# Delta rule: the state summed in PSUM and block-diagonal over both row halves, small row tiles for the other products, y turned by an identity

## The reference

```python
# attention by the delta rule: batch 4, heads 8, 768 tokens, head dim 48
k_n = k / (np.linalg.norm(k, axis=-1, keepdims=True) + 1e-06)
for t in range(S):
    y[:, :, t] = np.einsum('bhd,bhde->bhe', q[:, :, t], state)
    v_old = np.einsum('bhde,bhd->bhe', state, kt)
    state = state + bt * np.einsum('bhd,bhe->bhde', kt, vt - v_old)
# then two feed-forward layers over 3072 tokens, d_model 384, d_ff 2048
g = (a0 + a1*h + a2*h2 + a3*h3) / (1 + |b0|*|h| + |b1|*h2 + 1e-6)      # layer 1
g = h * tanh(softplus(h))                                            # layer 2
```

## Time and profile before

| | us |
|---|---|
| median of 3 runs | 1184.11 |
| lowest, highest | 1168.52, 1193.58 |
| the profiled execution | 1173.33 |
| its span, first to last instruction | 1171.5 |

### The profile page before, as it was taken

The page is one execution under the profiler, slowest core; times in us unless marked ns, Lnnn a source line. Parts: engine busy times, 40 slices in busy tenths (PEclk is TensorE's granted clock), DMA queues, the critical chain, the costliest instruction groups (busy, mean ns, idle before and its releaser), DMA issues.

```text
span 1171.5 us, 22278 instructions
## 1 busy us (share of the span) xinstructions
PE 1071.8 (91%) x9321; PEld 870.6 (74%) x9366; DVE 950.9 (81%) x1045; ACT 766.7 (65%) x1039; POOL 171.6 (15%) x328
## 2 busy tenths in 40 slices
PE   5388999999888899999999999889999999999997
PEld 3276877877766677787787777668888888888885
DVE  4965567554569999999999999999887888878785
ACT  1535456466367687777867768687676767667664
POOL 2088787780000000000000000000000000000000
PEclk7588889996899999999999999999999999999999
DMA  7625447343021010000101003230010101010000
GB/s 198 185 62 159 137 111 192 97 110 124 22 87 54 1 55 1 25 30 0 54 0 54 1 1 108 81 107 28 1 55 1 54 0 54 1 54 1 25 4 27
DMA packets 30489, 69.03 MB, mean 59 GB/s; under 512 B 4160, under 2 KB 11840, under 8 KB 30400
## 3 DMA queue, kind: packets, MB, share of 16 engines
q1 hardware_dynamic: 30144, 66.98, 19.2%
q10 hardware_dynamic: 256, 0.79, 0.3%
HBM read 53.60 MB, written 14.16 MB: 58 GB/s over the span
## 4 chain that ended last, share of the span: by engine, by line
DVE 35%; PE 33%; issue 3%; ACT 2%; DVEq 0%; ACTq 0%
PE o_ps L837 6%; PE o_ps L838 5%; PE o_ps L839 5%; PE h_ps L837 5%; PE h_ps L839 5%; PE h_ps L838 5%; DVE val L1022 5%; DVE val L1041 5%; DVE val L1054 5%; DVE g_lo L1060 5%; DVE den L1014 5%; DVE den L1049 5%; DVE pa L1020 4%; PE h_ps L881 0%; ACT den L901 0%
## 5 line engine op out<-in xcount | busy, mean ns | idle before, releaser
L910 ACT ACTIVATE g_hi<-val 128x1024 fp32r<-128x1024 f32 x96 | 102.0, 1062 | 99.7 <-DVE val L1054 93.6
L837 PE MATMUL o_ps<-g_hi,w_hi_late 128*128 128x512 f32 x288 | 116.8, 405 | 20.5 <-DVE g_lo L1060 20.4
L837 PE MATMUL o_ps<-g_hi,w_hi_early 128*128 128x512 f32 x288 | 114.8, 399 | 14.3 <-ACT stage L947 9.2
L1054 DVE SCALAR_TENSOR_TENSOR val<-den,val 128x1024 f32<-128x1024 f32 x96 | 117.7, 1226 | 10.7 <-DVE den L1049 0.5
L1060 DVE SCALAR_TENSOR_TENSOR g_lo<-val,g_hi 128x1024 fp32r<-128x1024 f32 x96 | 117.6, 1225 | 1.6 <-ACT g_hi L910 1.5
L837 PE MATMUL h_ps<-x_hi,w_hi_early 128*128 128x512 f32 x288 | 112.2, 390 | 2.0 <-DVE val L1022 2.0
L837 PE MATMUL h_ps<-x_hi,w_hi_late 128*128 128x512 f32 x288 | 112.5, 391 | 1.6 <-DVE w_lo_late L88 1.6
L838 PE MATMUL o_ps<-g_lo,w_hi_late 128*128 128x512 f32 x288 | 113.8, 395 | 0.0
L839 PE MATMUL o_ps<-g_hi,w_lo_early 128*128 128x512 f32 x288 | 113.5, 394 | 0.0
L838 PE MATMUL o_ps<-g_lo,w_hi_early 128*128 128x512 f32 x288 | 113.4, 394 | 0.0
L839 PE MATMUL o_ps<-g_hi,w_lo_late 128*128 128x512 f32 x288 | 113.3, 393 | 0.0
(11 more groups left out here) (111 smaller groups left out, 2360.2 us busy)
## 6 DMA issues: line engine op xcount, KB each, us to landing
w_raw<-w SPq DMA_DIRECT2D x16, 768.0 KB, 6.1
kv_run<-kv_n SPq DMA_DIRECT2D x24, 384.0 KB, 4.6
x_raw<-x_dram SPq DMA_DIRECT2D x12, 768.0 KB, 5.8
kq_run<-kq_t SPq DMA_DIRECT2D x44, 192.0 KB, 3.5
kq_gram<-kq_t SPq DMA_DIRECT2D x40, 192.0 KB, 6.7
x_dram<-stage SPq DMA_DIRECT2D x24, 192.0 KB, 4.0
x_dram<-stage SPq DMA_DIRECT2D x6, 768.0 KB, 4.3
out<-stage SPq DMA_DIRECT2D x5, 768.0 KB, 4.1
```

The source lines that it names most:

```text
L837: nc.tensor.matmul(dst, hi, rhs_hi, start=first, stop=False)
L910: act_fn(g_hi[:, n % 2], val[:, n % 2], ACT.Copy, scale=-1.0).then_inc(g_hi_ready, 1)
L1054: dve_stt(val[:, e], den[:, e], 2.0, val[:, e], ALU.subtract, ALU.mult).then_inc(g_ready, 1)
```

## The change

- **State.** It is no longer added up by DVE in SBUF. `update` adds in PSUM over the whole kernel (a start flag only for the first two steps), and the sum is copied to `state` after each step: the low row half by DVE (`copy_low`), the high by ACT (`copy_high`). `state` is block-diagonal over the two row halves, with zeros elsewhere.
- **k and q products.** Both use all 128 rows with 32 columns and 96 moving: 8 products each where there were 16. k and q of a turn are loaded once, into a ring of three turns, where they were loaded twice; the unused partitions are zeroed by POOL and, for turn 0, loaded by eight more transfers on ACT's queue (`load_pads`).
- **`solve` and `within`.** 16 products each of 32 rows, 32 columns and 48 moving, one for each head and batch, straight from `x_mat` and `p_mat`. `x_blk`, `p_blk` and `u_row` and the instructions that fill them go.
- **y.** It comes out by token; ACT copies it (`copy_y`), PE turns it with two products with an identity (`turn_y`, 96 columns, 128 moving) one step later, ACT copies it again (`copy_turned`).
- **keep_warm.** The two products in each step go. The burst of 12 stands ahead of every turn (before: turns 0 and 1), and PE waits ahead of it for that turn's inverse.
- **Order.** `weights(1)` moves behind the first inverse; `squares(tau + 3)` stands at s = 1 of turn tau on ACT, where squares(tau + 4) stood in chunk 2; `root_inverse` moves from s = 7 to s = 4; `turn_x` is always at s = 7.

```diff
-WARM = 2
-        kq_gram = sb("kq_gram", [P, CT, 2, G2 * V * B, C])
-        kq_run = sb("kq_run", [P, CT, 2, G2 * V * B, C])
+        kq = sb("kq", [P, RING * CT, 2, G2 * V * B, C])
...
+        def load_pads(q, c):
+            n = 2 * G2 * V * B * C
+            for r in range(HALVES):
+                q.dma_start(kq[64 * r + D:64 * r + 64, slot(0, c)].rearrange("p a s t -> p (a s t)"),
+                            kq_t[0, r][0:64 - D, c * n:(c + 1) * n]).then_inc(pads_loaded, 16)
...
             def k_state(tau, c, g):
-                pe.wait_ge(state_ready, q + 1)
+                pe.wait_ge(low_ready, q + 1)
+                if q >= 2:
+                    pe.wait_ge(high_ready, q - 1)
                 by_event()
-                for u, r, v in slots:
+                for v in range(V):
                     for b in range(B):
-                        s = B * v + b
-                        last = nc.tensor.matmul(ks_ps[quad(b), r, D * v:D * v + D],
-                                                kq_run[rows(r), c, 0, B * V * g + s],
-                                                state[rows(r), g, D * s:D * s + D], start=True, stop=True)
+                        at = HALVES * D * v
+                        last = nc.tensor.matmul(ks_ps[quad(b), at:at + HALVES * D],
+                                                kq[:, slot(tau, c), 0, B * (V * g + v) + b],
+                                                state[:, g, v, b].rearrange("p r d -> p (r d)"), start=True, stop=True)
...
             def solve(tau, c, g):
                 for u in range(U):
-                    last = nc.tensor.matmul(hz_ps[:, u], x_blk[:, c, U * g + u], z[:, g, u],
-                                            start=True, stop=True)
+                    for b in range(B):
+                        last = nc.tensor.matmul(hz_ps[quad(b), D * u:D * u + D],
+                                                x_mat[quad(b), tau % 2, HEADS * c + U * g + u],
+                                                z[quad(b), g, u], start=True, stop=True)
...
             def within(tau, c, g):
+                pe.wait_ge(q_done, q + 1)
+                by_event()
+                for v in range(V):
+                    for r in range(HALVES):
+                        for b in range(B):
+                            at = D * (HALVES * v + r)
+                            last = nc.tensor.matmul(y_bank[g][quad(b), at:at + D],
+                                                    p_mat[quad(b), tau % RING, HEADS * c + U * g + V * r + v],
+                                                    u_blk[quad(b), g, V * r + v, b],
+                                                    start=False, stop=True, skip_group_check=True)
+
+            def turn_y(q):
+                pe.wait_ge(y_copied, q + 1)
...
+                for r in range(HALVES):
+                    last = nc.tensor.matmul(turn_ps[0:V * D, P * r:P * r + P], y_tok[:, q % 2, r], ident[:],
+                                            start=True, stop=True)
...
             for tau in range(T):
                 for s in range(NQ):
...
-                    elif (tau, s) == (1, 0):
-                        pe.wait_ge(gram_used, 4 * (tau + 2))
-                        pe.wait_ge(inv_ready, 1)
+                    if tau and s == 0:
+                        pe.wait_ge(inv_ready, tau)
+                        if tau + 1 < T:
+                            pe.wait_ge(gram_used, 4 * (tau + 1) + 4)
                         by_event()
                         keep_warm(BURST)
-                    elif gram:
-                        pe.wait_ge(gram_used, 4 * (tau + 2) + fill)
-                        keep_warm(WARM)
                     solve(tau, c, g)
-                    if gram:
+                    if tau + 2 < T and 0 <= fill < 4:
                         gram_fill(tau + 2, fill)
                     q_state(tau, c, g)
...
+                    if q:
+                        turn_y(q - 1)
                     update(tau, c, g)
                     within(tau, c, g)
...
         def _(act):
+                    if q:
+                        copy_turned(q - 1)
+                    copy_high(tau, c, g)
+                    copy_y(tau, c, g)
+                    if c + 1 < CT:
+                        scale_v(tau, c + 1, g)
                     elif tau + 1 < T:
+                        scale_v(tau + 1, 0, g)
+                    if s == 1 and tau + 3 < T:
+                        squares(tau + 3)
...
         def _(dve):
-                dve_tt(u_row[:, g, 0:U * D].rearrange("p (u d) -> p u d", u=U), hz_ps,
-                       wgt[:, tau, cg:cg + U].unsqueeze(2).broadcast_to([P, U, D]), ALU.mult).then_inc(u_ready, 1)
-            def add_state(tau, c, g):
-                own = state[:, g, 0:V * B * D]
-                dve_tt(own, own, st_bank[g][:, 0:V * B * D], ALU.add).then_inc(state_ready, 1)
+            def copy_low(tau, c, g):
+                dve.wait_ge(st_done, index(tau, c, g) + 1)
+                nc.vector.tensor_copy(state[rows(0), g, :, :, 0], st_ps[g][rows(0)]).then_inc(low_ready, 1)
```

More of the change, by code:

```diff
@@ L188, in index, with slot, fill_of, bank_of @@
             return NQ * tau + G2 * c + g
-        slots = [(V * r + v, r, v) for v in range(V) for r in range(HALVES)]
+        def slot(j, c):
+            return CT * (j % RING) + c
+        def fill_of(bank):
+            return bank.rearrange("p (a c g v k) -> p a c g v k", a=2, c=2, g=G2, v=V)
+        def bank_of(j, f):
+            return early_banks[4 * j + f] if j < 2 else side_ps[:]
         STEPS = 2 * (C - 1)
-        def substitute(eng, tt, j, own, step, done):
-            for r in range(C - 1, 0, -1):
+        def rounds(eng, tt, j, own, step, done, first, last):
+            for r in range(first, last, -1):
                 shape = [P, r, C - r]
@@ L352, in gram_fill @@
                         for b in range(B):
-                            kq = operands[rows(r), 2 * cp + c2, :, B * s + b, :]
-                            last = nc.tensor.matmul(fill[quad(b), :, c2, s // V, s % V], kq[:, 0], kq,
+                            both = kq[rows(r), slot(j, 2 * cp + c2), :, B * s + b, :]
+                            last = nc.tensor.matmul(fill[quad(b), :, c2, s // V, s % V], both[:, 0], both,
                                                     start=True, stop=True)
                 last.then_inc(gram_done, 1)
-            def keep_warm(n):
-                for _ in range(n):
-                    nc.tensor.matmul(gram_bank[:], busy[:, 0:P], busy, start=True, stop=True)
             def k_state(tau, c, g):
@@ L455, in _ @@
                         k_state(tau + 1, 0, 0)
-                    if not gram:
-                        if tau + 2 < T and fill == 4:
-                            pe.wait_ge(gram_used, 4 * (tau + 2) + 4)
-                        keep_warm(WARM)
+                    if q:
+                        turn_y(q - 1)
                     update(tau, c, g)
                     within(tau, c, g)
+            turn_y(NQ * T - 1)
         @block.scalar
@@ new lines, in copy_high, with copy_turned @@
+            def copy_high(tau, c, g):
+                act.wait_ge(st_done, index(tau, c, g) + 1)
+                nc.scalar.activation(state[rows(1), g, :, :, 1], st_ps[g][rows(1)], ACT.Copy).then_inc(high_ready, 1)
+            def copy_turned(q):
+                tau, c, g = q // NQ, q % NQ // G2, q % G2
+                if c % 2 == 0 and g == 0:
+                    act.wait_ge(hand.y_stored[c // 2], 16 * tau + 16)
+                act.wait_ge(t_done, q + 1)
+                nc.scalar.activation(y_stage[0:V * D, :, g, P * c:P * c + P],
+                                     turn_ps[0:V * D, 0:HALVES * P].rearrange("p (r n) -> p r n", r=HALVES),
+                                     ACT.Copy).then_inc(t_copied, 1)
@@ L724, in _ @@
                         scale_gram(tau + 2, fill)
-                    add_state(tau, c, g)
+                    if s == (5 if tau == 0 else 4) and tau + 3 < T:
+                        root_inverse(tau + 3)
+                    copy_low(tau, c, g)
                     if (tau, s) == (0, 0):
```

357 lines of the change are left out of this document (160 added, 197 removed).

## The result

The changed kernel takes 1151.5 us (median of four runs, 1149.3 to 1156.6); the kernel before, beside it, 1176.3 (1168.1 to 1193.6). The ratio is 0.986, with a 95% interval of 0.982 to 0.991: faster by 1.4%, which the bound of 2% calls the same. The ratio is taken over fast runs alone, so it lies nearer to 1 than the quotient of the two medians, 0.979. The forecast was 1145 us, with a range of 1127 to 1185 and a chance of 0.64 for faster by more than 2%, 0.22 for a result in between. The profiled execution of the changed kernel is the slowest of its four, 1156.6 us (span 1154.8); that of before took 1173.3, so the two traces differ by 17 us where the medians differ by 25.

What follows compares the result with a forecast made beforehand. PE's own products were taken as the bound, with the clock and POOL setting the loop's end. Turns summed to an end at 291 us instead of 319.9: 29 less, 0.6 back, 1173.3 - 28 = 1145 us; range 1127 to 1185.

Steps and rivals of the forecast that it cites:

- 20 steps and 8 gram fills at 1.2 GHz: Turn 0, and turns 1 and 2 after two warm steps, at low clock: 4.8 us a step, 1.9 a fill.
- The step: One warm step of the loop: PE products of 2.35 us in sum, 2.8 us taken for it; bounds 2.5 and 3.3.
- priced: PE products: a record costs (2P + N) cycles of 2.4 GHz divided by tiles used in turn; good to about 20%.
- waits for PE to pass: Each step: more waits on PE (`y_copied`, `t_copied`, `q_done`, two for the state), the reason given for taking 2.8 us.
- Row tiles overlap: solve and within: four row tiles work at once, 11.7 ns a record, 0.37 us each; 47 ns without overlap.
- ACT's wait for squares: Turns 1 and 2: `squares(tau+3)` comes some 2.5 us late, PE stalls, and the rest of those turns runs at 1.2 GHz.
- Turn lengths: Six turns of the loop: 46 us for turn 0, 48 each for 1 and 2, then 31.6, 28 and 30; end at 291.
- POOL: Inverses on POOL: periods of 38.1 us, the last inverse ready at 261 us, ahead of turn 5.
- The clock staying low for lack of keep_warm: Rival, chance 0.15: without keep_warm the clock falls soon after each burst; loop ends at 354, 1208 us.
- Handovers that cost half a microsecond more: Rival, chance 0.15: waits PE meets with nothing queued make a warm step 3.3 us; loop ends at 312, 1167 us.
- Row tiles that take turns: Rival, chance 0.05: solve and within take 1.5 us each, a step 5.1; loop ends at about 349, 1203 us.
- POOL as the only bound: Rival, chance 0.20: the clock holds through most turns and each ends waiting for the inverse; loop ends at 279, 1133 us.

Runs made afterwards that it cites:

- wide kernel: Changed kernel with solve and within each as four products of 128 rows by 128 columns, computing something else; 1145.2 us, ratio to before 0.974.
- seventh: Changed kernel with turn_y in three column tiles of 32 instead of one of 96; 1154.9 us, ratio to before 0.989.
- eighth: Changed kernel with both turn_y and update in column tiles of 32; 1160.7 us, ratio to before 0.990.
- sixth: Changed kernel with squares(tau + 4) and its load moved back to chunk 2 of turn tau; 1151.9 us, ratio to before 0.987.
- third: Changed kernel with keep_warm's two products put back into each step; 1157.4 us, ratio to before 0.989.
- fourth: Changed kernel with the burst of 12 products only ahead of turn 0, the waits kept; 1152.2 us, ratio to before 0.982.
- the shifted one: Changed kernel with 128 events of PE's sequencer, no array work, added in the prologue; 1155.5 us, one run.

## Where the prediction was right and where it failed

**The number (partly luck).** The forecast of 1145 is 6.5 us under the median, and two errors stand against each other in it. It put 20 steps and 8 gram fills at 1.2 GHz, 111 us; a mean clock of 0.89 over 245 us comes to some 54 us at that level. And it put nothing for the supply of instructions, which stopped PE for 37 us inside groups.

**The step (right).** 2.35 us of products plus something for handovers gave 2.8; measured 3.02. The pieces: solve 0.45 from start to start (priced 0.37 without the border), q_state 0.35 (0.27), k_state 0.45 (0.27), turn_y 0.60 (0.53), update 0.81 (0.54), within 0.36 (0.37). What is over, 0.67 us, is not "waits for PE to pass" as the prediction had it but changes of the tile's shape. There are four in a step: solve to q_state 170 ns, k_state to turn_y 255, turn_y to update 309, update to within 415, where two groups of one shape follow each other in 22. The price goes with the moving columns of the product ahead of the change (48, 96, 128 and 192) and not with the shape that follows: behind update it is 415 ns with solve, within or the wide within next, and in the kernel before within (128 moving) to solve takes the same 309. The tile ahead counts as well: behind a solve of 128x128 tiles, 48 moving, it is 246 in the wide kernel and 247 in the kernel before, not 170. The seventh and eighth kernels take two of these away by making the shapes equal. By the Trainium skill (TensorEngine Tiling (Array Packing), Key Properties) a change of the tiling mode drains the array; the traces agree, and give the size.

**Row tiles overlap (right).** The 32 loads of solve or within start inside 0.30 us and their 32 matmuls inside 0.31 to 0.34, 10 to 11 ns from one to the next; priced were 11.7, and 47 if they had taken turns. The Trainium skill's rule that different row tiles can't use one PSUM bank at once (TensorEngine Tiling (Array Packing), Gotcha 1: PSUM Pressure) does not hold here for four diagonal tiles that write one bank.

**ACT's wait for squares (existed, worth nothing).** Twice, 2.9 us at most; forecast as 2.5 in turns 1 and 2 with a low clock for the rest of those turns, some 15 us each. The sixth kernel took it away and won nothing. The step that failed is the one from "DVE waits" to "PE stalls and the clock stays down": the clock in those turns was 0.93 and 0.89, and behind the two stalls looked at above it came back in some 6 us, not in 25 as in the earlier trace rows.

**Turn lengths (right in number for three, wrong in cause).** Forecast 46, 48, 48, 31.6, 28, 30; measured 47.2, 46.4, 44.9, 43.9, 33.3, 29.5. Turns 0 to 2 agree by accident. Turn 0 was to run at 1.2 GHz throughout; its clock was 0.78, and it had four stalls of 6.5 us. Turns 1 and 2 had not one long stretch at 1.2 GHz, but five stalls each. Turn 3 had no cause of slowness in the forecast, and was 12 us longer: in it four stalls, 6.8 us, and a clock of 0.84, which by my estimate costs some 7 us.

**The term that was missing.** The prediction counted array time, handovers, data, waits, the clock and POOL, but not how many instructions the new tiles need and how fast they must arrive. Inside groups that is 37 us over the loop (against 3 before), and falls of the clock stand behind some of it (the mean clock of the loop is 0.89, 0.86 before). Of the 245 us of the loop, 48 steps of 3.02 and 16 fills of 1.03 make only 161. This is where most of the gain went: the steps' own work became 48 x 1.16 = 56 us less and the loop 19 shorter, and of the 37 between them the stalls' growth is 34.

**POOL (period right, place wrong).** Its periods are 38 us, as read off, the last one 40; slow turns 2 and 3 gave it `n_turned` late, by 6.1 and 8.6 us. The forecast let the last turn wait for the last inverse, ready at 261. It was ready at 266.7, but PE ended turn 4 only at 269.6, so no wait for POOL stands there. The loop ended at 302 instead of 291 because turn 3 took 12 us more than forecast and turn 4 some 5 more, while turns 1 and 2 together took 5 less. These 11 us are what the forecast of 1145 missed in the trace (1156.6); against the median, 1151.5, it missed by 6.5.

**The rivals.** The clock staying low for lack of keep_warm: not so (third and fourth kernels). Handovers that cost half a microsecond more: 3.02 instead of 2.8 is less than half of that; its time, 1167, was not reached. Row tiles that take turns: not so, the step is 3.02 and not 5.1. POOL as the only bound: not reached, since PE got to the last turn after the inverse was ready.

**What stays open.** That the unit is a block of 256 instructions and 16 KB rests on the count of records between stalls (256.0, also with other events and products in it), on the queue's packets and on the shift by half a block. Stalls go with fetches that start late in their block; what makes a fetch start late isn't settled. The kernel before fetched 43 blocks in the loop with four stalls; that is one in 6.1 us, the changed kernel one in 4.9, the one with wide tiles one in 7.3, and no run fixes the density at which the supply begins to fail. Nor does a run tell how much of the time is the stalls and how much the clock: in the kernel with wide tiles both are gone together.

## What to carry to other kernels

When a large product is cut into small row tiles to save array time, count the instructions too: four times as many records at 10 to 11 ns each can be more than the supply delivers, and then PE stops in the middle of a group with "issue" as its only cause, the clock falls behind it, and here two thirds of what the products saved was lost. Look for waits of 1 us or more at a constant distance in instructions; if shifting the program by half a block moves them, it is the supply. Then fewer and wider products can be faster although the array works longer (here 53 us more of products, 6 us less of time), and products of one shape belong next to each other, as long as that doesn't take more instructions (the seventh and eighth kernels made the shapes equal with more of them, and gained nothing).

## What the runs showed of the hardware

- Stalls of the matrix engine, 0.6 to 4.7 us from load to load, at multiples of 125.5 weight loads, which with matmuls and events are 256 instructions; in the changed kernel each ends 2.2 to 2.8 us after a 16 KB packet of the instruction queue starts (up to 3.7 in the shifted one). They moved by 63 loads when 128 sequencer instructions were put ahead, and there was none inside a group with a fifth fewer instructions in the whole kernel.
- A change of the tile's shape costs from load to load 170, 255, 309 and 415 ns behind products of 48, 96, 128 and 192 moving columns, beside 22 between within and solve and 62 between q_state and k_state, which share a shape.
- Behind two idle times of PE, 1.79 and 1.30 us, in turn 3 the clock was 0.50 for about 6 us of dense products and returned without a burst; behind the one of 1.82 us in the earlier trace rows it stayed at 0.51 for 25 us. What makes the difference was not tried.
- Loads and matmuls on four 32x32 tiles of the diagonal, writing one PSUM bank, start every 10 to 11 ns on average (32 of either in 0.30 to 0.34 us).
